# Soft mixture of experts and a gated layer on one core: mixing-weight blocks, expert halves and the split of w_out put elsewhere

## The reference

```python
# 1: x = delta-rule recurrence over 768 steps for 4 x 8 heads of 48 (3072 tokens x 384)
# 2: soft mixture of experts, 8 experts x 4 slots
logits = x @ phi                                   # 3072 x 32
d = softmax of logits over tokens; slot_input = d.T @ x
slot_out[e] = np.maximum(slot_input[e] @ w1[e], 0.0) @ w2[e]     # 384 -> 1024 -> 384
c = softmax of logits over the 32 slots; x = c @ slot_out
# 3: gated layer, 384 -> 2048 -> 384
h = x @ w_in
g = h * (1.0 / (1.0 + np.exp(-1.702 * h)))
out = g @ w_out
```

## Time and profile before

| what | value |
|---|---|
| median of 3 runs | 526.88 us (525.96 to 527.99) |
| profiled execution, its own time | 527.37 us |
| its span in the profile | 525.5 us (so 1.87 us lie around it) |
| busy, share of the span | PE 87%, DVE 67%, ACT 59%, POOL 2% |
| mean granted TensorE clock | 0.958 |
| chain that ended last, by engine | PE 53%, ACT 20%, DVE 16%, issue 7%, DMA 3% |

### The profile page before, as it was taken

How to read it: one execution, slowest core, us unless ns; L and a number is a source line. 1 busy time by engine, 2 the same in 40 slices (tenths; PEclk the granted TensorE clock), 3 DMA queues, 4 the chain that set the end, 5 groups by cost and what they waited for, 6 DMA issues and landing times.

```text
span 525.5 us, 17657 instructions
## 1 busy us (share of the span) xinstructions
PE 456.1 (87%) x7296; PEld 335.6 (64%) x7296; DVE 353.0 (67%) x1177; ACT 311.8 (59%) x711; POOL 8.2 (2%) x20
## 2 busy tenths in 40 slices
PE   7548877878777788876999599999999999999997
PEld 4434655656555566554433277788888888888885
DVE  3798999999989986422651377656565666556653
ACT  2212788788878888777230356655655655655553
POOL 2000000000000000000000000000000000000000
PEclk9557899999999999989999799999999999999999
DMA  4911344666531233699999600010100100100101
GB/s 168 374 45 41 95 124 143 190 186 186 159 100 34 78 98 111 178 212 230 335 401 412 239 0 1 7 54 1 60 0 0 60 0 0 60 0 0 62 0 61
DMA packets 24295, 59.18 MB, mean 113 GB/s; under 512 B 3104, under 2 KB 11296, under 8 KB 23840
## 3 DMA queue, kind: packets, MB, share of 16 engines
q1 hardware_dynamic: 24224, 58.16, 34.6%
HBM read 53.43 MB, written 4.72 MB: 111 GB/s over the span
## 4 chain that ended last, share of the span: by engine, by line
PE 53%; ACT 20%; DVE 16%; issue 7%; DMA 3%; ACTq 0%; DVEq 0%
PE bank L815 10%; PE bank L817 10%; PE bank L816 10%; ACT zb L827 9%; PE bank L524 6%; ACT nv L870 4%; DVE tmp L1104 4%; DVE tt L1109 4%; PE bank L793 3%; DMA wo<-in_w_out 2%; DVE g_l L1316 2%; DVE g L1313 2%; PE bank L672 2%; ACT state L827 2%; ACT g_h L827 2%
## 5 line engine op out<-in xcount | busy, mean ns | idle before, releaser
L815 PE MATMUL bank<-g_h,wo_h 128*128 128x512 f32 x288 | 113.0, 392 | 2.3 <-DVE g_l L1316 2.1
L1316 DVE TENSOR_TENSOR g_l<-g,g_h 128x512 fp32r<-128x512 f32 x96 | 66.5, 693 | 71.5 <-ACT g_h L827 71.5
L817 PE MATMUL bank<-g_l,wo_h 128*128 128x512 f32 x288 | 112.1, 389 | 0.0
L816 PE MATMUL bank<-g_h,wo_l 128*128 128x512 f32 x288 | 112.1, 389 | 0.0
L827 ACT ACTIVATE g_h<-g 128x512 fp32r<-128x512 f32 x96 | 60.7, 633 | 77.6 <-DVE g L1313 77.6
L1109 DVE TENSOR_TENSOR tt<-tt,tmp 128x110 f32<-128x110 f32 (+35 forms) x366 | 75.1, 246 | 0.2
L1104 DVE TENSOR_TENSOR tmp<-nm,tt 128x110 f32<-128x110 f32 (+35 forms) x366 | 74.8, 245 | 0.2
L1313 DVE TENSOR_TENSOR g<-bank,sig 128x512 f32<-128x512 f32 x96 | 66.2, 689 | 11.2 <-ACT sig L993 6.0
L524 PE MATMUL bank<-zb,kn 128*32 128x192 f32 (+1 forms) x736 | 40.6, 334 | 38.0 <-ACT zb L827 37.5
L827 ACT ACTIVATE zb<-bank 32x192 f32<-32x192 f32 x192 | 61.6, 321 | 6.7 <-PE bank L510 4.6
L815 PEld LDWEIGHTS bank<-g_h,wo_h 128*128 128x128 f32 x288 | 54.0, 188 | 17.5 <-issue 5.7
(11 more groups left out here) (147 smaller groups left out, 448.8 us busy)
## 6 DMA issues: line engine op xcount, KB each, us to landing
kq<-in_kq_t SPq DMA_DIRECT2D x24, 512.0 KB, 4.0
slice<-in_w SPq DMA_DIRECT2D x28, 384.0 KB, 11.2
slice<-in_w SPq DMA_DIRECT2D x12, 512.0 KB, 3.7
slice<-in_w SPq DMA_DIRECT2D x24, 256.0 KB, 5.0
vn<-in_v_nat SPq DMA_DIRECT2D x24, 192.0 KB, 3.1
out_t<-res SPq DMA_DIRECT2D x18, 256.0 KB, 2.0
kn<-in_k_nat SPq DMA_DIRECT2D x23, 192.0 KB, 2.8
win<-in_w_in SPq DMA_DIRECT2D x3, 1024.0 KB, 15.4
```

What stands on the lines that cost most here:

```text
L815: eng.matmul(acc[d][:], wo_h[:, f, cols], g_h[:, f % GR], start=(f == 0), stop=False)
L816: eng.matmul(acc[d][:], wo_l[:, f, cols], g_h[:, f % GR], start=False, stop=False)
L817: i = eng.matmul(acc[d][:], wo_h[:, f, cols], g_l[:, f % GR], start=False, stop=(f == NF - 1))
L1316: eng.tensor_tensor(g_l[:, f % GR], g[:, f % GR], g_h[:, f % GR].bitcast(F32), ALU.subtract).then_inc(s_gl, 1)
```

## The change

Five edits. (1) A half of an expert's slice is now all 128 partitions and half of the columns. (2) The six `c_block`s leave the first matmuls of the experts: blocks 0 and 1 stand around `slots_turned(1)`, 2 and 3 ahead of M's part 1, 4 and 5 ahead of its part 2; `c_out` follows on both engines, with other banks, and `c_l` has a place of its own, since `hid1` is now written earlier. (3) `m_h` and `m_l` stand ahead of the first split of `w_out`. (4) `w_out` is split tile by tile: tiles 0 and 1 before the blocks, tile f + 2 in tile f of block 0. (5) TensorE begins h for two tiles before M's last part, and a tile f < 15 of every block now takes its six products with g_h first and waits for g_l only before the last three.

```diff
@@ load_expert_half
-                rows = slice(64 * h, 64 * h + 64)
-                eng.dma_start(w_slices[i][rows, q], weights_of(i, q)[rows]).then_inc(s_w[i], DMA)
+                n = w_slices[i].shape[2] // 2
+                cols = slice(n * h, n * h + n)
+                eng.dma_start(w_slices[i][:, q, cols], weights_of(i, q)[:, cols]).then_inc(s_w[i], DMA)
@@ tensor
-            CB = (bk[3], bk[4], bk[6], bk[7], bk[3], bk[4])
+            CB = (bk[3], bk[2], bk[0], bk[1], bk[3], bk[2])
...
-            hidden(0, 0)
-            hidden(0, 1)
-            c_block(0)
-            c_block(1)
-            c_block(2)
-            hidden(0, 2)
-            c_block(3)
+            for kt in range(KT):
+                hidden(0, kt)
             hidden(1, 0)
-            c_block(4)
-            c_block(5)
             hidden(1, 1)
-
-            eng.wait_ge(a_co, 3)
-            eng.wait_ge(v_co, 3)
             hidden_turned(0)
             hidden(1, 2)
             out(0, 0)
...
             slots_turned(0)
             for j in range(1, W2):
                 out(1, j)
+
+            c_block(0)
             slots_turned(1)
+            c_block(1)
             eng.wait_ge(v_sot, NEG)
             for k in range(KT):
+                if k:
+                    c_block(2 * k)
+                    c_block(2 * k + 1)
                 eng.wait_ge(s_win[k], DMA)
...
             for i in range(NMB - 1):
                 m_rests(i)
-            m_heads(NMB - 1)
-            m_rests(NMB - 1)
...
+            eng.wait_ge(a_co, 3)
+            eng.wait_ge(v_co, 3)
             for f in range(LEAD):
                 h(0, f)
+            m_heads(NMB - 1)
+            m_rests(NMB - 1)
...
                     if first:
-                        eng.wait_ge(v_wo, wo_rows(f)[1] + 1)
+                        eng.wait_ge(v_wo, f + 1)
                     eng.wait_ge(s_gh, per_ff(k, NF, f + 1))
-                    eng.wait_ge(s_gl, per_ff(k, NF, f + 1))
+                    if f == NF - 1:
+                        eng.wait_ge(s_gl, per_ff(k, NF, f + 1))
                     for d in range(KT):
...
                         eng.matmul(acc[d][:], wo_l[:, f, cols], g_h[:, f % GR], start=False, stop=False)
-                        i = eng.matmul(acc[d][:], wo_h[:, f, cols], g_l[:, f % GR], start=False, stop=(f == NF - 1))
                         if f == NF - 1:
-                            i.then_inc(s_acc, 1)
-                        elif d == KT - 1:
-                            i.then_inc(s_use, 1)
+                            eng.matmul(acc[d][:], wo_h[:, f, cols], g_l[:, f % GR], start=False, stop=True).then_inc(s_acc, 1)
+                    if f < NF - 1:
+                        eng.wait_ge(s_gl, per_ff(k, NF, f + 1))
+                        for d in range(KT):
+                            i = eng.matmul(acc[d][:], wo_h[:, f, P * d:P * d + P], g_l[:, f % GR], start=False, stop=False)
+                        i.then_inc(s_use, 1)
@@ scalar
-            c_out(0, bk[3], 1)
-            c_out(2, bk[6], 3)
             c_head(1)
...
             def hidden(g, bank):
                 eng.wait_ge(p_h, KT * (g + 1))
+                if g:
+
+                    eng.wait_ge(v_cl, 2)
...
             turned(1)
-            split_w_out(0)
+            c_out(0, bk[3], 1)
+            c_out(2, bk[0], 3)
+            c_out(4, bk[3], NCA + 2)
             eng.wait_ge(p_m, 1)
             copy(m_h[:], bk[7][:]).then_inc(a_mh, 1)
+            split_w_out(0)
             m_out(0)
-            m_out(2)
...
-            for f in range(LEAD):
-                sigmoid(0, f)
-                g_head(0, f)
+            sigmoid(0, 0)
+            m_out(2)
+            g_head(0, 0)
+            split_w_out(1)
+            sigmoid(0, 1)
+            g_head(0, 1)
...
-                    if first and f + FPP < NF:
-                        split_w_out(f + FPP)
+                    if first and f + LEAD < NF:
+                        split_w_out(f + LEAD)
@@ vector
-            split_w_out(0)
+            c_out(1, bk[2], 2)
+            c_out(3, bk[1], 4)
+            c_out(5, bk[2], NCA + 4)
             eng.wait_ge(a_mh, 1)
             eng.tensor_tensor(m_l[:], bk[7][:], m_h[:].bitcast(F32), ALU.subtract).then_inc(v_ml, 1)
+            split_w_out(0)
             m_out(1)
-            m_out(3)
...
-            for f in range(LEAD):
-                tile(0, f)
+            tile(0, 0)
+            m_out(3)
+            split_w_out(1)
+            tile(0, 1)
```

More of the change, by code:

```diff
@@ L167, in program @@
         logits = at("logits", FRONT + 9, [P, NT, NS])
+        c_l = at("c_l", FRONT + 9, [P, NT * C], F32R)
         c_stack = at("c_stack", FRONT, [P, N], F32R)
@@ L204, in program @@
         ct = st("ct", 51, [P, NT, C])
-        c_l = st("c_l", 51, [P, NT * C], F32R)
         c_h = st("c_h", 54, [P, NT * C], F32R)
@@ L285, in wo_part @@
             return t[:, FPP * i:FPP * (i + 1)]
-        def wo_rows(f):
-            return (slice(0, FPP) if f < FPP else slice(f, f + 1)), max(f - FPP + 1, 0)
         HALVES = ((0, 1), (2, 3))
@@ L711, in c_block @@
                     eng.wait_ge(v_sel, 1)
-                if i == 2:
-                    eng.wait_ge(f_lo, NGT)
                 if i in (0, NCA):
@@ L964, in split_w_out @@
             def split_w_out(f):
-                rows, _ = wo_rows(f)
                 eng.wait_ge(s_wo[f // FPP], DMA)
-                if f == FPP:
-                    eng.wait_ge(p_o, NEG * W2)
-                copy(wo_h[:, rows], wo[:, rows]).then_inc(a_wo, 1)
+                copy(wo_h[:, f], wo[:, f]).then_inc(a_wo, 1)
             def m_out(i):
@@ L976, in _ @@
             hidden(0, bk[1])
-            c_out(4, bk[3], NCA + 2)
             turned(0)
@@ L1255, in _ @@
             c_rest(0)
-            c_out(1, bk[4], 2)
             c_sums(1)
             c_turned(1)
-            c_out(3, bk[7], 4)
             c_rest(1)
@@ L1279, in split_w_out @@
             def split_w_out(f):
-                rows, n = wo_rows(f)
-                eng.wait_ge(a_wo, n + 1)
-                eng.tensor_tensor(wo_l[:, rows], wo[:, rows], wo_h[:, rows].bitcast(F32), ALU.subtract).then_inc(v_wo, 1)
+                eng.wait_ge(a_wo, f + 1)
+                eng.tensor_tensor(wo_l[:, f], wo[:, f], wo_h[:, f].bitcast(F32), ALU.subtract).then_inc(v_wo, 1)
             def m_out(i):
@@ L1288, in _ @@
             hidden(0, bk[0])
-            c_out(5, bk[4], NCA + 4)
             turned(0)
```

## The result

The changed kernel takes 525.13 us (median of 22 runs), the kernel before 526.64 us beside it (22 runs). The ratio of the undisturbed runs is 0.9961, with a 95% interval of 0.9943 to 0.9979: 0.39% or some 2 us faster (the medians differ by 1.5 us), where 3.6 us were forecast.

The account below looks back on a forecast made before the run. Bounds: recurrence and TensorE until 280 us, `wo`'s load and w_out's split before m_l, VectorE and ScalarE in block 0, then TensorE. -6.5 + 2.0 + 0.2 + 0.6 = -3.7, taken as -3.6 from 526.88: 523.3 us, range 520.9 to 526.1.

Parts of the forecast that it names:

- clearly faster: Whole kernel: a time below 524.25 us, some 0.5% under the kernel before; chance 0.66.
- rival C: Expert loads: column halves load no faster, M still ends at 291.94, total 525.0 us; chance 0.14.
- three signs of being wrong: A slice or `win` waited for before M; ScalarE waiting for `wo` behind m_h; block 0 not paced by VectorE.
- Step 1: Expert loads: column halves reach 400 GB/s, slices 7 and later start some 3 us earlier, `win` lands 287.6 to 289.0.
- Step 2: Experts: without the c_blocks they save 2.90 us, their last product ends at 283.34.
- Step 3: M with the moved c_blocks: takes 6.9 us and ends at 290.25, not 291.94, 1.7 us less.
- Step 4: Behind M: m_h ahead of w_out's split, at full clock, brings g of tile 0 6.5 us earlier.
- B: Around M's end: TensorE falls to half clock all the same, 1.0 us less gain, 524.3 us; chance 0.17.
- Step 5: Block 0: splitting w_out tile by tile lengthens VectorE's way by 2.0 us.
- Step 6: Block ends: products with g_l last cost 0.15 us at each of four, 0.6 together, and 0.2 at block 0's.
- E: Block 0: TensorE's fresh start behind v_wo in every tile makes it the bound, 531.8 us; chance 0.06.
- D: Moved c_blocks overlap neighbours and block ends cost nothing, 1.0 and 0.6 us better, 521.7 us; chance 0.08.

Follow-up runs that it names:

- 1: The kernel before with only the expert halves cut by columns; 527.51 us, ratio 0.9976 to the kernel before.
- 2: The changed kernel with the expert halves cut by partitions (rows) again; 527.07 us, ratio 0.9963 to the kernel before.
- 6: The kernel before with only the c_blocks and their copies moved into the waits of M; 527.74 us, ratio 1.0023.
- 11: The changed kernel with the c_blocks back among the experts' first matmuls; 525.13 us, ratio 0.9970 to the kernel before.
- 3: The kernel before with only m_h and m_l put ahead of the four-tile split of w_out; 525.23 us, ratio 0.9911.
- 9: The changed kernel with w_out's first four tiles split in one instruction again, behind m_h and m_l; 524.09 us, ratio 0.9945 to the kernel before.
- 4: The changed kernel with the old product order and the wait for g_l at each tile's head; 524.09 us, ratio 0.9904 to the kernel before.
- 10: As 7, with the w_out pieces one tile earlier and m_out(3) in a wait for g_h; 517.73 us, ratio 0.9804 to the kernel before.
- 7: As 5, with tile 0 of blocks 1 to 5 in the old product order; 520.93 us, ratio 0.9872 to the kernel before.
- 8: As 5, with all tiles in the old product order; 521.86 us, ratio 0.9905 to the kernel before.
- 5: The changed kernel with the w_out piece between g and g_l on VectorE, ahead of the sigmoid on ScalarE; 521.24 us, ratio 0.9895 to the kernel before.

## Why the prediction came half true

The bounds were read rightly: ScalarE's order behind M, VectorE's pace in block 0, and the banks at the ends of blocks are where the time went and came from. Of 3.7 us of gain 2.2 came. The outcome held the likelier, clearly faster (0.66), didn't. The time is next to rival C's 525.0 us, but C isn't what happened, as the column halves did load faster: that nearness is chance. Of the prediction's three signs of being wrong two came: a slice was waited for before M (0.62 us), and ScalarE waited for `wo` behind m_h (0.28 us, which cost nothing). By its own steps:

- **Step 1** is a term of the sum that was mis-sized. Its mechanism holds: no backlog stands, the column halves move 326 GB/s at full share where the others moved 236. But "slices 7 and later start some 3 us earlier" was 1.3 us. From issue to full rate took 3.4 us where I had put 2, and the issue itself came 0.2 us late against t0 (249.56 - 258.36 where 250 - 259.02 was assumed), as a part of SyncE's time is waiting for places and not for bandwidth. The last part of `win` landed near 289.0 (issued at 272.1, 16.9 us to landing), 30.6 us behind t0; forecast were 28.6 to 30.0 (and the early bound, 3 us under 290.87, should have been 287.9 and not 287.6). What the edit is worth stays open: 0.75 us alone (1) and 0.55 inside the change (2) are both within the scatter of M's end. The price of rival C, 1.7 us for "no faster", was too high in any case: with the halves by rows (2) M ended 0.54 us later, held by slice 13 and not by `win`. The Trainium skill's rule in "SBUF — State Buffer", "Door 1: The DMA port swizzle", that 64 neighbouring partitions reach half of the ports, agrees in direction with 236 against 326 and 399 GB/s, which are ratios of 0.72 and 0.59. The Trainium skill's wish for at least 1 MiB a load in "DMA: Bandwidth & Descriptors", "Rules for kernel authors", shows little here: loads of 384 KB moved 399 GB/s, those of 1 MB 410 to 421, those of 768 KB only 372.
- **Step 2** failed in "TensorE never waited for a slice", which I carried over to a TensorE that comes 2.9 us earlier. The experts ended 24.7 us behind t0 instead of 24.3, after 0.62 us of waiting, and up to 1.73 us where the halves are rows (6). Moving the blocks was summed at 1.7 us; the runs show 0.26 us in the change (11) and nothing alone (6), neither to be told from scatter.
- **Step 3**: M took 7.1 us from the experts' end, 6.9 were summed. With step 2's 0.4 its end came 0.64 us late against t0: 1.05 us earlier than before, not 1.7, and the scatter of M's end is as large.
- **Step 4** was right in its mechanism and carries the change. From M to g 8.48 us became 3.99, and three runs divide the 4.49 us: 3.05 for m_h and m_l ahead of the split (3), 0.69 from there to 9, by the place of m_out(3), and 0.75 for the smaller piece (9). 3.7 us were expected; the 0.3 lie between m_stack and the first sigmoid (292.23 to 293.59, 1.36 instead of 1.0). The clock held at 1.00, so B did not happen in the profiled execution; but in 3, 4 and 10, which also have m_h ahead, the clock fell at the start of block 0.
- **Step 5** was exact, 2.02 us for 2.0, and the pace stayed at 2.46. What I had not asked is what the split bought in return: 0.75 us (9). It should have been a term of step 4 with a sign against step 5.
- **Step 6** was too small: 1.28 us for 0.8, or 1.2 by the difference that 4, 7 and 8 show. One product more behind the copy at the end of block 0 is 0.23 us, as summed; the other four ends cost about 0.25 each instead of 0.15, since TensorE not only waits 0.1 but starts afresh (0.34 us to the next product instead of 0.23).

So of the 1.46 us that are missing, 0.64 are M's end (steps 1 to 3), 0.3 step 4 and 0.48 step 6.

E did not happen: VectorE set the pace all through block 0. Nor did D: the moved blocks are no denser than summed, and the ends cost more.

What stays open: the ratios of 3, 4 and 10 (-4.7, -5.1 and -10.3 us) (1 less the ratio, times 527) are larger than their stretches (-2.6, -3.4 and -7.0), and for 3 and 10 the stretches lie just outside the intervals (-6.3 to -3.1 and -12.9 to -7.7). The stretches are of one execution each and leave out all that lies ahead of t0, and the profiled execution of before had a high clock: its mean was 0.958, while the executions of that kernel beside 1 to 4 had 0.951 in the median and those beside 9 to 11 had 0.954. Over the 22 executions of the change, 0.01 less of mean clock goes with 3.1 us more time (a fitted line, correlation -0.76). By that, an estimate, the clock accounts for some 2 us of the difference in 3 and 4 and over 1 us in 10. The rest is not explained.

Nor is it settled why the clock fell in 10 and not in 9. It need not be the kernel: in the recurrence, whose instructions are the same in all, the mean clock was 0.83 from 130 to 150 us in 11 and 0.86 from 160 to 170 in 2, and 1.00 in both stretches in the change. One trace of each kernel can't tell what belongs to the kernel and what to the execution.

## What to carry to other kernels

Ask of every piece of preparatory work which wait it could fill: behind g_l the piece `wo_l` made VectorE's pace 2.46 us a tile, while between g and g_l, where the engine waited 0.70 us for another one, it was 2.29, with TensorE's own at 2.27, and this is what the best kernel is made of. When work leaves a stage that loads are racing with, the gain is cut off at the next load, so read how far ahead each load is (here 0.5 to 1.7 us short) before counting it. Split a stretch at the point where its cause changes: s1 as a whole gave edit 3 a gain of 3.9 us, of which 0.85 was a load that landed earlier by chance. And in an accumulation over several banks, count the products that stand between two banks' first uses: with two in place of three, each block's end had a stall of 0.2 us that no average shows.

## What the runs showed of the hardware

- TensorE's clock fell to 0.50 near the start of block 0 in some kernels and not in others with almost the same instructions. In the kernel before it was low from 294 to 301 us, in 1 and 6 around the same place and again from 302 or 301 on, in 3, 4 and 10 from 297, 298 and 295 on; in the change and in 2, 5, 7, 8, 9 and 11 it stood at 1.00 there. In 1, 3 and 6 block 0 was 0.5, 1.4 and 0.6 us longer with the fall inside it; in 10 it missed its expectation by 1.3. In 3 it followed rests of 1.23 and 2.27 us with one product between, in 4 one of 1.32; but in 10 the two microseconds ahead of it were busy for 1.07, while in 9 there were two such pairs in a row (1.16 and 1.00) and it held, as it did in 8 after two microseconds with 0.49.
- The mean granted clock of one kernel differs between executions: 0.950 to 0.967 in the 22 of the change, and their times go from 527.67 to 521.46 us, the lower clocks with the longer times.
- Loads of all 128 partitions in pieces of 192 and 256 KB moved 326 GB/s at full share of the DMA engines (238 / 0.73, an estimate), those of 384 KB 399 to 408, those of 1 MB 410 to 421 (281 to 287 us) and those of 768 KB 372 (290 to 293 us), halves of 64 partitions 236.
- From the issue of the first slice to full rate took 3.4 us, in a queue that was not empty.
- Slice 13 landed up to 1 us earlier or later between executions of kernels with the same loads: the wait for it was 0.62, 0.66, 0.74, 0.81, 1.37, 1.64 and 0.49 us in the change, 4, 5, 7, 8, 9 and 10.
